# Second layer's weight combinations rounded and split on GpSimd alone, with six staging blocks

## The reference, cut to what matters

```python
def _moe_ref(x, w_in, w_out):                 # first feed-forward layer
    h = x @ w_in                              # 4608x512 @ 512x2048
    g = np.maximum(0.01 * h, h)
    return (g @ w_out).astype(np.float32)

def _moe2_ref(x, w_in, w_out):                # second feed-forward layer
    h = x @ w_in
    relu6 = np.clip(h + 3.0, 0.0, 6.0)
    g = h * relu6 / 6.0
    return (g @ w_out).astype(np.float32)

def reference(**kwargs):
    ...
    attn_out = _attn_ref(**attn_kwargs)       # 8 batches, 8 heads, 576 tokens; keys pooled by 8
    ...
    x = _moe_ref(x=x, **moe_kwargs)
    return _moe2_ref(x=x, **moe2_kwargs)
```

## Time and profile before

| what | value |
|---|---|
| median of 3 runs | 1778.17 us (1777.17 to 1780.1) |
| the profiled execution, its own time | 1781.4 us |
| its span | 1779.6 us |
| TensorE matmul busy | 1731.9 us, 97% |
| VectorE busy | 890.3 us, 50% |
| ScalarE busy | 663.4 us, 37% |
| GpSimd busy | 452.9 us, 25% |
| mean DMA rate | 144 GB/s |

### The profile page before, as it was taken

How to read it: one execution, slowest core, us unless ns; L and a number is a source line. 1 busy time by engine, 2 the same in 40 slices (tenths; PEclk the granted TensorE clock), 3 DMA queues, 4 the chain that set the end, 5 groups by cost and what they waited for, 6 DMA issues and landing times.

```text
span 1779.6 us, 28996 instructions
## 1 busy us (share of the span) xinstructions
PE 1731.9 (97%) x9642; PEld 1487.1 (84%) x9642; DVE 890.3 (50%) x1498; ACT 663.4 (37%) x1233; POOL 452.9 (25%) x548
## 2 busy tenths in 40 slices
PE   7899999999999999998979999999999999999999
PEld 7787888888888888886768889889988998998898
DVE  8555565565565554552222244454545454545444
ACT  3544333333333333333444234343434343343332
POOL 7553222222222121213754312130303031211200
PEclk7899999999999999999999999999999999999999
DMA  5332112122122112114557786666656575656562
GB/s 171 113 118 78 51 59 87 41 82 65 42 79 65 56 65 75 46 45 160 198 197 261 256 277 190 212 196 197 219 183 219 171 225 176 222 172 224 176 196 76
DMA packets 141548, 255.41 MB, mean 144 GB/s; under 512 B 14528, under 2 KB 22720, under 8 KB 141504
## 3 DMA queue, kind: packets, MB, share of 16 engines
q1 hardware_dynamic: 141504, 254.86, 44.5%
HBM read 203.42 MB, written 51.38 MB: 143 GB/s over the span
## 4 chain that ended last, share of the span: by engine, by line
PE 82%; DVE 7%; ACT 3%; POOL 3%; issue 2%; DMA 2%; SPq 0%; DVEq 0%; ACTq 0%; POOLq 0%
PE ps_h L1247 14%; PE ps_y L1183 13%; PE ps_y L1185 13%; PE ps_y L1184 13%; PE ps_att L1247 6%; PE ps_h L1183 6%; PE ps_h L1185 6%; PE ps_h L1184 5%; PE ps_att L1183 2%; DVE gate L999 2%; POOL prep_sum L674 2%; PE ps_att L1184 1%; PE ps_att L1185 1%; POOL prep_stage L681 1%; PE ps_att L1327 1%
## 5 line engine op out<-in xcount | busy, mean ns | idle before, releaser
L1247 PE MATMUL ps_h<-xs_hi,ring 128*128 128x256 f32 x1440 | 301.1, 280 | 1.4 <-DVE u L1049 1.1
L1247 PEld LDWEIGHTS ps_h<-xs_hi,ring 128*128 128x128 f32 x1440 | 240.1, 188 | 14.0 <-issue 2.1
L1183 PE MATMUL ps_h<-x_hi,win_hi 128*128 128x512 f32 x576 | 233.6, 406 | 12.9 <-DVE gate L999 12.9
L1183 PE MATMUL ps_y<-g_hi,wout_hi 128*128 128x512 f32 x576 | 231.1, 401 | 4.5 <-DVE g_lo L1002 4.5
L1184 PE MATMUL ps_h<-x_lo,win_hi 128*128 128x512 f32 x576 | 228.7, 397 | 0.0
L1185 PE MATMUL ps_h<-x_hi,win_lo 128*128 128x512 f32 x576 | 228.7, 397 | 0.0
L999 DVE TENSOR_TENSOR gate<-ps_h,pre 128x512 f32<-128x512 f32 x144 | 99.1, 688 | 257.2 <-ACT pre L787 256.2
L1185 PE MATMUL ps_y<-g_hi,wout_lo 128*128 128x512 f32 x576 | 227.7, 395 | 0.0
L1184 PE MATMUL ps_y<-g_lo,wout_hi 128*128 128x512 f32 x576 | 227.4, 395 | 0.0
L1185 PE MATMUL ps_y<-wout_hi,g_lo 128*128 128x512 f32 x576 | 227.3, 395 | 0.0
L1183 PE MATMUL ps_y<-wout_hi,g_hi 128*128 128x512 f32 x576 | 226.8, 394 | 0.0
(11 more groups left out here) (134 smaller groups left out, 3115.0 us busy)
## 6 DMA issues: line engine op xcount, KB each, us to landing
ring<-w_in_split SPq DMA_DIRECT2D x504, 256.0 KB, 2.7
w_in_split<-prep_stage SPq DMA_DIRECT2D x56, 256.0 KB, 2.1
k_raw<-in_kT SPq DMA_DIRECT2D x32, 288.0 KB, 2.9
q_raw<-in_qT SPq DMA_DIRECT2D x32, 288.0 KB, 4.1
v_raw<-in_v SPq DMA_DIRECT2D x32, 288.0 KB
x0T<-x_stage SPq DMA_DIRECT2D x32, 288.0 KB, 2.1
x1T<-y_stage SPq DMA_DIRECT2D x36, 256.0 KB, 2.1
x_stage<-x1T SPq DMA_DIRECT2D x36, 256.0 KB, 3.7
```

The lines of the kernel that those rows point to most:

```text
L1183: pe.matmul(acc, left[0], right[0], start=first, stop=False)
L1247: mm = pe.matmul(banks[BANK_OF[r]], a, b[:, r, c, :], start=r < 3 and c == 0 and n == 0, stop=c == 1 and n == 2, skip_group_check=True)
```

## The change

The rounding copies of the preparation move from ScalarE to GpSimd, which now does both halves of each split (`prep_split`, `prep2_split`). `PREP_STAGES` goes from 3 to 6, the separate buffer `prep_stage2` goes, and the row blocks of `w_out` use three double slots of `prep_stage`. ScalarE's `tile` loses the placement of these copies.

```diff
-PREP_STAGES = 3
+PREP_STAGES = 6
...
-            def prep_lo(i, k):
+            def prep_split(i, k):
                 n = PRODUCTS * i + PREP_ORDER.index(k)
                 stage = prep_stage[:, n % PREP_STAGES]
+                if k in (S1, S2, S3, S4):
+                    pool.wait_ge(s_summed, 4 * i + (S1, S2, S3, S4).index(k) + 1)
+                if n >= PREP_STAGES:
+                    pool.wait_ge(prep_stored[n % PREP_STAGES], 16 * (n // PREP_STAGES))
+                nc.gpsimd.tensor_copy(stage[:, 0:2], prep_source(i, k)).then_inc(prep_hi_ready, 1)
                 pool.wait_ge(prep_hi_ready, n + 1)
                 nc.gpsimd.tensor_tensor(stage[:, 2:4], prep_source(i, k),
                                         stage[:, 0:2].bitcast(F32), ALU.subtract
                                         ).then_inc(prep_lo_ready, 1)
-            def prep2_lo(e):
+            def prep2_split(e):
+                pool.wait_ge(raw_loaded[e % 2], 64 * HF // 2 + 16 * (e // 2 + 1))
+                slot = e % (PREP_STAGES // 2)
+                if e < PREP_STAGES // 2:
+                    for n in (2 * slot, 2 * slot + 1):
+                        pool.wait_ge(prep_stored[n], stores_of(n))
+                else:
+                    pool.wait_ge(prep2_stored[slot], 16 * (e // (PREP_STAGES // 2)))
+                nc.gpsimd.tensor_copy(prep2_stage(e)[:, 0], raw_row(e)).then_inc(prep_hi_ready, 1)
                 pool.wait_ge(prep_hi_ready, HF * PRODUCTS + e + 1)
-                nc.gpsimd.tensor_tensor(prep_stage2[:, e % 2, 1], raw_row(e),
-                                        prep_stage2[:, e % 2, 0].bitcast(F32), ALU.subtract
+                nc.gpsimd.tensor_tensor(prep2_stage(e)[:, 1], raw_row(e),
+                                        prep2_stage(e)[:, 0].bitcast(F32), ALU.subtract
                                         ).then_inc(prep_lo_ready, 1)
...
-                    if prep == 1 and place % HF < PRODUCTS:
-                        prep_hi(place // HF, PREP_ORDER[place % HF])
-                    if prep == 2 and place % 2 == 0 and place < 2 * FC:
-                        prep2_hi(place // 2)
...
-            tile(ATT_TILES, False, prep=1)
-            tile(TILES - 1, False, prep=2, last=True)
+            tile(ATT_TILES, False)
+            tile(TILES - 1, False, last=True)
```

More of the change, by code:

```diff
@@ L218, in ffn_attention_kernel @@
             sb("prep_raw", [P, 2, 4, 2, P]), sb("prep_sum", [P, 4, 2, P]),
-            sb("prep_stage", [P, PREP_STAGES, 4, P], F32R),
-            sb("prep_stage2", [P, 2, 2, N], F32R)))
-        prep_raw, prep_s, prep_stage, prep_stage2 = prep
+            sb("prep_stage", [P, PREP_STAGES, 4, P], F32R)))
+        prep_raw, prep_s, prep_stage = prep
         xs_hi = sb("xs_hi", [P, PRODUCTS, 2, HN], F32R)
@@ L302, in ffn_attention_kernel @@
         prep_stored = [sem(f"prep_stored{i}") for i in range(PREP_STAGES)]
-        prep2_stored = [sem(f"prep2_stored{i}") for i in range(2)]
+        prep2_stored = [sem(f"prep2_stored{i}") for i in range(PREP_STAGES // 2)]
         ring_loaded = [sem(f"ring_loaded{i}") for i in range(RING)]
@@ L346, in prep_source, with prep2_stage, stores_of @@
                     S2: prep_s[:, 1], S3: prep_s[:, 2], S4: prep_s[:, 3]}[k]
+        def prep2_stage(e):
+            slot = e % (PREP_STAGES // 2)
+            return prep_stage[:, 2 * slot:2 * slot + 2].rearrange("p a b f -> p a (b f)")
+        def stores_of(n):
+            return 16 * len(range(n, HF * PRODUCTS, PREP_STAGES))
         def raw_row(e):
@@ L479, in store_prep2 @@
                 sp.wait_ge(prep_lo_ready, PRODUCTS * HF + e + 1)
-                sp.dma_start(w2_out_split[e], prep_stage2[:, e % 2].bitcast(F32)
-                             ).then_inc(prep2_stored[e % 2], 16)
+                sp.dma_start(w2_out_split[e], prep2_stage(e).bitcast(F32)
+                             ).then_inc(prep2_stored[e % (PREP_STAGES // 2)], 16)
             def load_ring(i, r):
@@ L578, in _ @@
             for e in range(PREP_STAGES):
-                sp.wait_ge(prep_stored[e], 16 * len(range(e, HF * PRODUCTS, PREP_STAGES)))
-            for e in range(2):
-                sp.wait_ge(prep2_stored[e], 16 * FC // 2)
+                sp.wait_ge(prep_stored[e], stores_of(e))
+            for e in range(PREP_STAGES // 2):
+                sp.wait_ge(prep2_stored[e], 16 * len(range(e, FC, PREP_STAGES // 2)))
             for i in range(2):
@@ L756, in _ @@
                 for k in PREP_ORDER:
-                    prep_lo(i, k)
+                    prep_split(i, k)
             for e in range(FC):
-                prep2_lo(e)
+                prep2_split(e)
             pool.wait_ge(h_done, FC * (TILES - 1) + 3 * BLOCKS)
@@ L801, in copy_y @@
                                          ).then_inc(y_copied_act, 1)
[L803 to L821, removed]
             def x_hi2(t, r):
@@ L826, in x_hi2 @@
                     for e in range(PREP_STAGES):
-                        act.wait_ge(prep_stored[e], 16 * len(range(e, HF * PRODUCTS, PREP_STAGES)))
-                    for e in range(2):
-                        act.wait_ge(prep2_stored[e], 16 * FC // 2)
+                        act.wait_ge(prep_stored[e], stores_of(e))
+                    for e in range(PREP_STAGES // 2):
+                        act.wait_ge(prep2_stored[e],
+                                    16 * len(range(e, FC, PREP_STAGES // 2)))
                 else:
@@ L933, in stage, with tile @@
                                          ACT.Copy, scale=V_SCALE).then_inc(x0_copied, 1)
-            def tile(T, attention, last=False, pieces={}, prep=0):
+            def tile(T, attention, last=False, pieces={}):
                 for place in range(4 * FC):
```

## The result

The changed kernel was timed in three rounds of measurement, each beside the kernel before on the same chip:

| round | changed | before | ratio (95% interval) |
|---|---|---|---|
| first | 1770.39 us (6 runs) | 1778.24 | 0.9960 (0.9945 to 0.9975) |
| second | 1768.39 us (5 runs) | 1778.67 | 0.9939 (0.9925 to 0.9952) |
| third | 1770.34 us (6 runs) | 1778.98 | 0.9958 (0.9944 to 0.9973) |

What follows compares the result with a forecast made beforehand. TensorE, 97% busy, was held by late ScalarE chains in tiles 7 and 8, 24.9 us at most; late ring loads and the DMA queue left a gain of 17.9, so 1778.2 - 17.9 = 1760.3 us, range 1752.5 to 1773.

Steps and rivals of the forecast that it cites:

- What bounds the kernel and what goes: Tiles 7 and 8: TensorE waits for late ScalarE chains, which stand 40.9 us for stores; these waits and clock loss go.
- What can be had: Tiles 7 and 8: 204.05 us elapsed against 179.2 undisturbed, so at most 24.9 us to gain.
- The price of the cast: GpSimd's rounding cast, placed between memset and select: 0.40 us for 256 columns, 0.70 for 512.
- 74 us per us: Tiles 7 and 8: effect of a change in cast price, 56 times in tile 7 and about 2 x 9 in tile 8.
- Stretching by VectorE: GpSimd in tile 7: operations stretched once or twice a step, 1.0 us per step, 8 in all.
- The rival in which GpSimd becomes the bound: Cast as dear as a subtraction (0.74, 1.29): ring loads at 1002, 1785 us; decides from 0.64 on; chance 0.11.
- The loop of tile 8: Row-block loop set by store issue, load issue and landing, 3.62 us: 5.68 us a pair, ring loads at 977.0.
- What is late next: Second layer's loads: full DMA queue makes TensorE wait 4 us for group 2, then until 1016.1 for the ring.
- Nothing further is lost: After step 2's start: later ring blocks need 0.7 us of DMA where a part takes 1.4, so no more loss.
- The sum: Whole kernel: gain of 17.9 us from the median of 1778.2, giving 1760.3 us.
- Complete cover: Rival: ring loads early enough, or the DMA queue passes step 2's blocks sooner; 1753.3 us, chance 0.14.
- A lock between GpSimd and VectorE: Rival: g_lo stops GpSimd up to 11 us in tile 7; adds 3 us, 5 at most: 1763 to 1765.

Runs made afterwards that it cites:

- The two halves: Each half of the change alone: six slots with copies on ScalarE, 1769.36 us; both split parts on GpSimd with three slots, 1771.51 us.
- prefetch: Changed kernel with four raw row blocks of w_out in flight in place of two: 1759.08 us, ratio 0.9880 to the kernel before.
- reorder: Changed kernel with step 2's ring loads issued ahead of w_out group 3 and the y store, groups ordered 0, 2, 1: 1767.16 us, ratio 0.9930.
- The fastest version: Changed kernel with four raw row blocks in flight and step 2's ring loads ahead of group 3 and the y store: 1753.16 us, ratio 0.9856.
- the x_hi2 moved: Changed kernel with ScalarE's seven x_hi2 of tile 8 placed behind the last chain: 1770.02 us, ratio 0.9947.
- the row blocks first: Changed kernel with loads of the first two w_out row blocks ahead of the y stores and the second layer's first input: 1767.97 us, ratio 0.9930.

## Why the prediction was wrong

**What bounds the kernel and what goes: right.** TensorE's waits in tile 7 for `gate` and `g_lo` are gone, the clock is 1.00 through it. The two halves show what did it: ScalarE must not wait for a store ahead of a chain, and either more slots or another engine for the copies sees to that. With more slots alone the first raw block of each tile still costs TensorE 9.6 us; with the copies on GpSimd it does not.

**What can be had: a little more than I said.** I took 5.60 us a block from two rows of tile 8 and got 24.9 us. That pace was that of one execution's tile 8: 0.2333 us a matmul, where the changed kernel has 0.2289 and 5.49 a block. Undisturbed, two tiles take 175.8 us (measured with prefetch and reorder together), and 28 us could be had in that profile. The fastest version gained 25.8 between medians.

**The price of the cast: right.** 0.40 forecast, 0.40 measured; 0.61 instead of 0.70 for 512 columns. The Trainium skill's 769 ns for 512 elements in a one-input loop (GPSIMD Engine Reference, Performance versus the Vector engine) is above the 0.61; the measurement decides. My sentence that by it the result would be about 2 us later does not follow from the prices beside it: 0.07 us on the 18 casts of tile 8 is 1.3 us, and 74 us per us would make 5.2. Stretching by VectorE was about as taken: with it the mean of the casts of 256 columns is 0.42 us from prep_raw and 0.49 from prep_sum, a step took 12.39 us (823.39 to 922.49 in eight) for 12.2. The rival in which GpSimd becomes the bound by its price falls with it.

**The loop of tile 8: the term that was mis-sized.** I took 3.62 us from one load of before, and 5.68 a pair. The first three pairs took 6.49, 6.25 and 6.17 us: the loads took 4.06 and 3.89 us to land, and subtractions and casts were stretched (1.82 for 1.29). The seven pairs took 41.65 us where I had 39.8, and the last block came 2.86 behind the one before it where I had 2.0. The first cast came at 931.87 instead of 930.4, which is the 1.4 us by which tile 7's preparation ended late. Together they put the ring loads at 981.27 instead of 977.0; over the four profiles the mean is 981.0, 4.0 us late. Prefetch, which takes the loads out of this chain, brought the gain over before to 20.0 us, some 11 more than the change alone.

**What is late next: right in place and size.** 38.2 us between ring loads and step 2 was the forecast (1015.2 - 977.0). Measured: 38.5, 37.65, 38.1 and 38.8 in the changed kernel, 37.8 with the x_hi2 moved, 38.2 with the prefetch, 38.25 with the row blocks first. Waits of 4 us for group 2 and again before step 2 came as described. The wait on ScalarE in tile 8, which I had half expected to be absorbed, was, and the move of x_hi2 shows it.

**"Nothing further is lost" was the second error.** From the start of step 2 to TensorE's last matmul the kernel before takes 742.9 us in all four profiles, the changed one 743.0, 744.6, 743.0 and 745.8: 1.2 more on average. In the fourth profile the window behind the wait reads

```profile
1016.00:1024.00 8.00, 5.42 (x22) 4.65 (x22) 1.41 (x4) 1.57 (x3) 0.00 (x0) 0.66 1.05 397
1024.00:1032.00 8.00, 8.00 (x47) 7.11 (x47) 2.64 (x6) 1.11 (x2) 5.11 (x4) 0.91 1.06 387
```

against 1.00 in both windows of the first. A wait of 3 us before step 2 was followed by nothing in two profiles and by 1.7 and 2.9 us of lost time in the others, and I had priced the wait alone, although showed the effect.

**The sum.** 17.9 less 4.0 (ring loads) less 1.2 (clock) is 12.7. The first profile of before had 219.4 us from tile 7 to step 2 where the mean of its four is 218.1 (218.1, 218.8 and 216.0 for the others): 1.3 less. That gives 11.4, and the means of the profiles differ by 11.5. The timed medians differ by 7.9, 10.3 and 8.6. The 1 to 4 us that are left between the profiles and the medians are open: single executions of one kernel spread by 4 to 10 us within a round, profiled ones are not shown to be different, and four of each do not fix a mean to better than about 1.5 us.

**The rivals.** Complete cover (1753.3 us) did not happen to this change, but is what prefetch and reorder together reach, at 1753.16. A lock between GpSimd and VectorE is in the trace: in the first profile 25 of GpSimd's sums, casts and subtractions of tiles 7 and 8 took over 0.05 us longer than their usual time, and each of the 25 overlaps `g_lo` or `x_lo`, VectorE's operations with two inputs in SBUF; of the 40 that overlap only `gate`, which has one of its inputs in PSUM, none is stretched (22 more overlap `g_lo` and are not stretched either). The other three profiles show the same. In tile 7 the stretching adds up to 8.5 us, near the 8 in my sum and under the 11 of this rival, so little of its 3 us was lost there. The trace agrees with the Trainium skill's rule (SBUF — State Buffer, Who interferes with whom); no experiment took the overlap away.

## What to carry to other kernels

When a stall ahead of a stage boundary goes, look for the queue that the next stage's loads form: the gain is at most the smaller of the stall and the slack of those loads, and here 38 us of queued bytes fixed the start of step 2 in every version that kept the order of the loads and reached it early. An engine's free time is no measure for a loop that goes through DMA: in tile 8 it was load latency, not GpSimd, that set the loop, while in tile 7 GpSimd's added casts delayed the loop's start. Two more buffers in memory already there gained some 11 us on top of the change and nothing without it: which edit pays depends on what has gone before it. Take a pace or a latency from several rows, and price the clock behind every new wait.

## What the runs showed of the hardware

- A GpSimd cast from float32 to float32r takes 0.40 us for 128x256 and 0.61 for 128x512, slope 0.8 ns a column, the slope of its memset; a subtraction with the same output takes 0.74 and 1.29.
- At a granted clock of 1.00 two paces of the same matmul occur: 0.2289 and 0.2333 us, the latter in stretches of 5 to 54 us after waits (850 to 892 and 936 to 990 us in the first profile of before; 830 to 856 in its fourth), and not after every wait. What decides it stays open.
- While the DMA engines are fully busy (share 1.05, 387 GB/s, 996 to 1004 us in the changed kernel), SyncE itself is held while issuing: 4.63 us for one load of 1 MB at 999.67, where one issued at 1001.15 in the kernel before, in a window with a share of 0.58, takes 0.36.
- A GpSimd operation that reads SBUF was stretched only beside a VectorE operation with two inputs in SBUF: 25 of 25 stretched ones in tiles 7 and 8 of the changed kernel's first profile (0.86 for 0.40 in a cast, 1.82 for 1.29 in a subtraction), and none of 40 beside `gate`, which has one input in PSUM.
